# Attention output: every second product with v copied out of PSUM by ScalarE and its halves added by GpSimd

## The chip, the core and the metric

The kernel runs on one core of a Trainium2 chip. The core has four engines that compute: TensorE (PE in the profile; matrix products into PSUM), VectorE (DVE), ScalarE (ACT) and GpSimd (POOL). SyncE (SP) starts most of the transfers from and to HBM. Each engine works through its own list of instructions in order, and waits on counters (semaphores) that the other engines raise. The metric is the time in microseconds from the first to the last instruction of one execution and what lies around it; lower is better.

## The reference

Attention with a mask by clusters, over 2 x 8 = 16 heads of 768 rows and 64 columns, and two layers after it over the 1536 rows that come out:

```
mask   = argmax(q_n @ c_n.T)[:, None] == argmax(k_n @ c_n.T)[None, :]      # per head, 16 centroids
scores = where(mask, q @ k.T / 8, -1e9)
attn   = softmax(scores)
x      = attn @ v                      # 16 heads, put side by side: 1536 x 512
h      = x @ w_in                      # 1536 x 2048
g      = (a0 + a1 h + a2 h^2 + a3 h^3) / (1 + |b0||h| + |b1|h^2 + 1e-6)
x      = g @ w_out                     # 1536 x 512
out    = (silu(x @ w_gate) * (x @ w_val)) @ w_out2
```

Everything is float32. The kernel gets this precision from TensorE by splitting each operand into a high and a low part, and adding the products of the parts.

## The kernel before

The attention is written as a list of steps, and every engine runs the same list. A step holds the work of several tiles at different stages. A tile is 128 query rows of one head against its 768 keys, so a head has six tiles and there are 96. At step s:

- TensorE computes the scores of tile s (lines 1226 and 1229), turns the finished probabilities of tile s-5 (six transposes, line 1239, into PSUM banks 4 and 5, in two halves of three), and then makes a third of a product with v (lines 1254 and 1256). It also has the small products that find the clusters of a later head: the transposes of line 1278 and the product of line 1292 in two neighbouring steps of a head, and line 1313 in the next two.
- ScalarE takes the exponential of tile s-1 (line 811), and copies the transposed probabilities of tile s-5 out of PSUM, rounded to the high part, in two halves (line 829).
- VectorE takes the row maximum of tile s (line 1035), and subtracts the high part of tile s-5 from what stands in PSUM, again in two halves, which gives the low part (line 1057). TensorE may write the next tile's transposes into those two banks only after that: the first three wait for the first half of the subtraction of the tile before, the second three for its second half (lines 1236 to 1238).
- GpSimd divides three finished tiles by their row sums every third step (line 589). TensorE transposes them after that. It splits q, k and v of later heads (lines 597 to 617), parts of the first layer's weights (lines 624 and 626), and x (lines 636 and 638).

A product with v is made per group. A group is half a head, that is three tiles or 384 query columns, and there are 32 of them, numbered g. The high and the low part of v stand side by side as weights. So of the result in bank 6 (O_BANK) 64 partitions hold the product with the high part, and the other 64 that with the low part; for every second head the two are swapped by choosing r = 0 or 64, so that two heads fill the 128 partitions of x. The two have to be added. Before the change this is done in the step in which the product ends, last on both engines: ScalarE copies one half to x_part (line 839), and VectorE adds the other, straight from PSUM, to give x_raw (line 1066). TensorE begins the next group's product in the next step, after its transposes, and waits there for that addition (line 1251). When a pair of heads is complete, GpSimd waits for the additions and splits x into x_hi and x_lo.

Below, the steps of a head are counted 0 to 5. The product of an even group (g = 0, 2, ...) ends in step 4, that of an odd group in step 1. Step 4 is also the one in which line 1278 stands on TensorE, behind the product with v; line 1292 is in step 5, and line 1313 in steps 0 and 1. GpSimd has the split of a pair of heads at the end of its step 0, in every second head. Heads are numbered h = 0 to 15, and h holds groups 2h and 2h+1; h odd has r = 64.

After the last tile TensorE goes on without a pause with the first layer, in units n of 12 + 12 products of 512 columns, in which GpSimd multiplies once (line 516).

Of the kernel before, what the change touches and what calls it, by code (L numbers as in the profile page):

```python
# [21 lines left out]
def build_program(nc, q, k, v, centroids, w_in, w_out1, a, b, w_gate, w_val, w_out2, out):  # L22
# [44 lines left out]
    def at(name, shape, dt, offset):  # L67
        return nc.alloc_sbuf_tensor_at(name, shape, dt, offset=offset)
# [17 lines left out]
    x_lo = at("x_lo", [P, DC, NTOK], F32R, X_AT + X_BYTES)  # L86

    x_raw = at("x_raw", [P, DC, NTOK], F32, X_AT + X_BYTES)

# [125 lines left out]
    def sem(name):  # L215
# [4 lines left out]
    s_v_in = [sem(f"s_v_in{i}") for i in range(2)]  # L220
    s_vhi, s_vlo, s_logit_lo, s_logit_sum, s_xpart, s_xsum = (sem(x) for x in (
        "s_vhi", "s_vlo", "s_logit_lo", "s_logit_sum", "s_xpart", "s_xsum"))
    s_copy = [sem(f"s_copy{i}") for i in range(3)]
# [14 lines left out]
    s_pT, s_pT_hi, s_pT_lo, s_pv, s_xhi, s_xlo = (sem(x) for x in (  # L238
        "s_pT", "s_pT_hi", "s_pT_lo", "s_pv", "s_xhi", "s_xlo"))
    s_w1p_hi, s_w1p, s_w1hi, s_w1lo = (sem(x) for x in ("s_w1p_hi", "s_w1p", "s_w1hi", "s_w1lo"))  # L240
    s_w2sum, s_w2hi, s_w2lo, s_wohi, s_wolo = (sem(x) for x in (
# [122 lines left out]
    with block:  # L364
# [114 lines left out]
        def _(pool):  # L479
# [103 lines left out]
            for step in STEPS:  # L583
# [47 lines left out]
                if third == HALF - 1 and g1 % 4 == 3:  # L631
                    pool.wait_ge(s_xsum, g1 + 1)
                    finish_last()
                    h = g1 // 2
                    xh, xl, raw = x_pair(x_hi, h), x_pair(x_lo, h), x_pair(x_raw, h)
                    did(g.tensor_scalar(xh, raw, 1.0, 1.0, ALU.mult, ALU.mult), s_xhi)
                    pool.wait_ge(s_xhi, h // 2 + 1)
                    did(g.tensor_tensor(xl, raw, xh.bitcast(F32), ALU.subtract), s_xlo)
                    finish_last()
# [18 lines left out]
        def _(sc):  # L658
# [144 lines left out]
            for step in STEPS:  # L803
# [30 lines left out]
                if third == HALF - 1:  # L834
                    r = (g // 2) % 2 * D
                    sc.wait_ge(s_pv, g + 1)
                    if g:
                        sc.wait_ge(s_xsum, g)
                    s.activation(x_part[r:r + D, :], ps[D - r:P - r, O_BANK, 0:HC], ACT.Copy
                                 ).then_inc(s_xpart, 1)  # L840
                if head_at(step, S_CEN) == 0:
# [32 lines left out]
        def _(ve):  # L874
# [136 lines left out]
            for step in STEPS:  # L1011
# [49 lines left out]
                g, third = pv_at(step)  # L1061
                if third == HALF - 1:

                    ve.wait_ge(s_xpart, g + 1)
                    r = (g // 2) % 2 * D
                    v_.tensor_tensor(x_of(x_raw, g), ps[r:r + D, O_BANK, 0:HC],
                                     x_part[r:r + D, :], ALU.add).then_inc(s_xsum, 1)
# [31 lines left out]
        def _(pe):  # L1099
# [40 lines left out]
            def first_result(n):  # L1140
                u = n % NF1
                pe.wait_ge(s_glo, n + 1)
                if n == 0:
                    pe.wait_ge(s_pT_lo, 2 * NT)
                    pe.wait_ge(s_xsum, NG)
                for d in range(DC):
                    if u == 0 and n:
                        pe.wait_ge(s_yraw, (n // NF1 - 1) * DC + d + 1)
                    w = slice(DM + d * P, DM + (d + 1) * P)
                    last = three(ps[:, RES + d, :], w1_hi[u][:, w], w1_lo[u][:, w], g_hi[n % 3][:, :],  # L1150
                                 g_lo[n % 3][:, :], u == 0, u == NF1 - 1)
                last.then_inc(s_y, 1)
# [57 lines left out]
            for step in STEPS:  # L1210
# [33 lines left out]
                if g is not None:  # L1244

                    h = g // 2
                    if third == 0:
                        pe.wait_ge(s_pT_lo, T * (g + 1))
                        pe.wait_ge(s_vlo, h + 1)
                        if g:  # L1250
                            pe.wait_ge(s_xsum, g)
                    for kt in (2 * third, 2 * third + 1):
# [124 lines left out]
```

## Time and profile before

| | |
|---|---|
| three timed runs | 794.4, 795.75 and 795.83 us, median 795.75 |
| the profiled execution's own time | 794.28 us |
| its span, first to last instruction | 792.5 us |
| TensorE busy | 781.2 us (99%) |
| VectorE busy | 571.9 us (72%) |
| GpSimd busy | 522.7 us (66%) |
| ScalarE busy | 517.3 us (65%) |
| granted TensorE clock, mean | 0.996 |

The span is the time from the first to the last instruction of one execution that the hardware profiler took. The attention steps lie from about 20 to 262 us of it, and the two layers after that. A timeline row gives the start, the duration, the engine, the line, what is written and read, and the number of instructions merged into the row; the brackets give the idle time of the engine just before, and what ended it. Short gaps have no bracket. Ends of products on TensorE are modelled: each row of them looks longer than the time until the next one starts, so starts are compared here and not ends.

### The profile page before, as it was taken

The page shows a single profiled execution, that of the slowest core. Times are in us where ns is not written, and L with a number is a line of the kernel's source. Part 1 is how long each engine was busy: PE and PEld are TensorE (multiplying, and loading weights), DVE is VectorE, ACT ScalarE, POOL GpSimd, SP SyncE. Part 2 cuts the span into 40 slices and gives each one's busy share as a digit, 9 for nine tenths or more (in the row PEclk, how much of TensorE's full clock was granted, in tenths as well). Part 3 has the DMA queues.
Part 4 walks back from the last instruction along what each step waited for, and adds up shares of the span by engine and source line. Part 5 has one row for each costly group of instructions (what it writes and reads, how often), then busy time and mean ns, then how long its engine had stood idle before and what let it go on. Part 6 is the DMA issues. An engine that isn't in the chain of part 4 may idle for free.

```text
span 792.5 us, 12617 instructions
## 1 busy us (share of the span) xinstructions
PE 781.2 (99%) x4204; PEld 697.7 (88%) x4204; DVE 571.9 (72%) x1043; ACT 517.3 (65%) x957; POOL 522.7 (66%) x457
## 2 busy tenths in 40 slices
PE   8999999999999999999999999999999999999998
PEld 7799999999998888888888888899999999999997
DVE  5899999999997888778777777745445545554453
ACT  4888888888887787777767889744444444333322
POOL 4767988998575799322222288888889876655620
PEclk8999999999999999999999999999999999999999
DMA  8776555454310700000000011241111114111102
GB/s 206 180 199 162 143 140 125 116 145 121 85 60 19 221 28 0 1 1 1 1 1 0 1 55 54 66 147 50 32 54 53 37 45 134 54 28 53 28 1 80
DMA packets 57681, 57.92 MB, mean 73 GB/s; under 512 B 6608, under 2 KB 44304, under 8 KB 57616
## 3 DMA queue, kind: packets, MB, share of 16 engines
q1 hardware_dynamic: 57376, 56.52, 26.6%
q8 instruction: 34, 0.56, 0.3%
q10 hardware_dynamic: 240, 0.59, 0.3%
q14 instruction: 31, 0.25, 0.1%
HBM read 33.59 MB, written 3.15 MB: 46 GB/s over the span
## 4 chain that ended last, share of the span: by engine, by line
PE 87%; DVE 8%; issue 2%; ACT 2%; DMA 0%; DVEq 0%; ACTq 0%
PE ps L1111 18%; PE ps L1109 18%; PE ps L1110 18%; PE ps L1239 6%; PE ps L1204 4%; PE ps L1205 4%; PE ps L1203 4%; DVE neg_max L1035 3%; DVE probT_lo L1057 3%; PE ps L1254 3%; PE ps L1226 3%; PE ps L1256 3%; PE ps L1313 2%; PE ps L1229 2%; ACT prob L811 1%
## 5 line engine op out<-in xcount | busy, mean ns | idle before, releaser
L516 POOL TENSOR_TENSOR den<-den,mag 128x512 f32<-128x512 f32 x48 | 62.3, 1298 | 121.8 <-ACT den L689 121.6
L1111 PE MATMUL ps<-x_hi,w_lo 128*128 128x512 f32 (+1 forms) x384 | 139.5, 363 | 0.0
L1109 PE MATMUL ps<-x_hi,w_hi 128*128 128x512 f32 (+1 forms) x384 | 139.4, 363 | 0.0
L1110 PE MATMUL ps<-x_lo,w_hi 128*128 128x512 f32 (+1 forms) x384 | 139.3, 363 | 0.0
L575 POOL TENSOR_TENSOR w_lo<-w_raw,w_hi 128x768 fp32r<-128x768 f32 (+1 forms) x48 | 101.6, 2125 | 56.4 <-ACT w_hi L742 56.4
L589 POOL TENSOR_SCALAR prob<-prob,row_inv 128x768 f32<-128x768 f32 x96 | 85.6, 907 | 39.2 <-DVE row_inv L1049 38.7
L829 ACT ACTIVATE probT_hi<-ps 128x384 fp32r<-128x384 f32 x192 | 84.2, 489 | 25.9 <-PE ps L1239 24.2
L1057 DVE TENSOR_TENSOR probT_lo<-ps,probT_hi 128x384 fp32r<-128x384 f32 x192 | 96.8, 545 | 5.3 <-ACT probT_hi L829 4.0
L1035 DVE TENSOR_REDUCE neg_max<-ps 128x1 f32<-128x768 f32 x96 | 91.1, 950 | 8.8 <-PE ps L1229 8.5
L811 ACT ACTIVATE prob<-ps,neg_max 128x768 f32<-128x768 f32 x96 | 86.8, 905 | 10.8 <-DVE neg_max L1035 10.1
L1239 PE MATMUL ps<-ident,prob 128*128 128x128 f32 x576 | 81.7, 277 | 4.4 <-DVE probT_lo L1057 4.1
L1239 PEld LDWEIGHTS ps<-ident,prob 128*128 128x128 f32 x576 | 65.6, 140 | 17.0 <-issue 9.9
L1109 PEld LDWEIGHTS ps<-x_hi,w_hi 128*128 128x128 f32 x384 | 72.1, 188 | 8.2
L1110 PEld LDWEIGHTS ps<-x_lo,w_hi 128*128 128x128 f32 x384 | 72.1, 188 | 8.2
L1111 PEld LDWEIGHTS ps<-x_hi,w_lo 128*128 128x128 f32 x384 | 72.1, 188 | 7.5
L1111 PE MATMUL ps<-g_hi,w_lo 128*128 128x512 f32 x192 | 74.8, 390 | 0.0
L1110 PE MATMUL ps<-g_lo,w_hi 128*128 128x512 f32 x192 | 74.8, 390 | 0.0
L1109 PE MATMUL ps<-g_hi,w_hi 128*128 128x512 f32 x192 | 74.8, 390 | 0.0
L1254 PE MATMUL ps<-probT_hi,v_split 128*128 128x384 f32 x192 | 72.5, 378 | 0.0
L763 ACT ACTIVATE act_hi<-ps 128x384 fp32r<-128x384 f32 x48 | 23.6, 492 | 64.6 <-DVE ps L992 43.7
L1256 PE MATMUL ps<-probT_lo,v_split 128*128 128x384 f32 x192 | 64.6, 337 | 0.0
L959 DVE TENSOR_TENSOR sum<-ps,gate 128x384 f32<-128x384 f32 x24 | 13.4, 557 | 68.9 <-PE ps L1111 68.9
(145 smaller groups left out, 1987.5 us busy)
## 6 DMA issues: line engine op xcount, KB each, us to landing
k_hihi<-qk_hi SPq DMA_DIRECT2D x32, 192.0 KB, 4.0
w_raw<-in_moe_w_gate SPq DMA_DIRECT2D x48, 128.0 KB, 2.3
w_raw<-in_moe_w_val SPq DMA_DIRECT2D x48, 128.0 KB, 2.5
w_raw<-in_moe_w_in SPq DMA_DIRECT2D x16, 256.0 KB, 3.7
w_raw<-in_moe_w_out SPq DMA_DIRECT2D x16, 256.0 KB, 5.0
qk_raw<-in_q SPq DMA_DIRECT2D x16, 192.0 KB, 3.4
q_hilo<-qk_hi SPq DMA_DIRECT2D x16, 192.0 KB, 3.4
qk_low<-qk_hi SPq DMA_DIRECT2D x16, 192.0 KB, 4.5
```

What stands on the lines that cost most here:

```text
L575: did(g.tensor_tensor(lo[:, wave, :], raw[:, wave, :], hi[:, wave, :].bitcast(F32), ALU.subtract), s_w2lo)
L589: did(g.tensor_scalar(prob[i][:, :], prob[i][:, :], row_inv[:, i:i + 1], 1.0, ALU.mult, ALU.mult), s_norm)
L811: s.activation(prob[i % T][:, :].rearrange("p (c n) -> p c n", c=2), ps[:, bank:bank + 2, 0:HC], ACT.Exp, bias=neg_max[:, i % T:i % T + 1] ...
L829: s.activation(probT_hi[g % 2][:, n * HALF:(n + 1) * HALF, c:c + P], ps[:, PT_BANK + n, 0:HC].rearrange("p (k n) -> p k n", k=HALF), ACT.C ...
L1035: v_.tensor_reduce(neg_max[:, i % T:i % T + 1], ps[:, bank:bank + 2, 0:HC], AX.XY, ALU.max, negate=True).then_inc(s_max, 1)
L1057: v_.tensor_tensor(probT_lo[g % 2][:, keys, c:c + P], ps[:, PT_BANK + n, 0:HC].rearrange("p (k n) -> p k n", k=HALF), probT_hi[g % 2][:, k ...
L1109: mm(dst, hi, m_hi, start=start, stop=False)
L1110: mm(dst, hi, m_lo, start=False, stop=False)
L1111: return mm(dst, lo, m_hi, start=False, stop=stop)
L1239: last = transpose(ps[:, PT_BANK + n, kt % HALF * P:(kt % HALF + 1) * P], prob[i % T][:, kt * P:(kt + 1) * P], ident[:, :])
L1254: mm(ps[:, O_BANK, 0:HC], vv, probT_hi[g % 2][:, kt, :], start=(kt == 0), stop=False)
L1256: last = mm(ps[:, O_BANK, 0:HC], vv, probT_lo[g % 2][:, kt, :], start=False, stop=(kt == T - 1))
```

## The change

The groups with an even number take another way out of PSUM. ScalarE makes two copies, one of each half: the first straight to x_low, a new name for the memory in which x_hi will stand later, the second to x_raw. VectorE does nothing for these groups. TensorE waits for the second copy (s_xmain) before the next product. When GpSimd splits a pair of heads, it first adds the two for the even groups of both heads in one instruction, 128 partitions by 384 columns, waits for that, and then splits as before. Odd groups go as they did, with counters that count half as far.

```diff
+    x_low = at("x_low", [P, DC, NTOK], F32, X_AT)
...
                 if third == HALF - 1 and g1 % 4 == 3:
-                    pool.wait_ge(s_xsum, g1 + 1)
+                    h = g1 // 2
+                    pool.wait_ge(s_xmain, h + 1)
+                    pool.wait_ge(s_xsum, h + 1)
                     finish_last()
-                    h = g1 // 2
                     xh, xl, raw = x_pair(x_hi, h), x_pair(x_lo, h), x_pair(x_raw, h)
+                    did(g.tensor_tensor(raw[:, 0:HC], raw[:, 0:HC], x_pair(x_low, h)[:, 0:HC], ALU.add), s_xboth)
+                    finish_last()
                     did(g.tensor_scalar(xh, raw, 1.0, 1.0, ALU.mult, ALU.mult), s_xhi)
...
                     sc.wait_ge(s_pv, g + 1)
-                    if g:
-                        sc.wait_ge(s_xsum, g)
-                    s.activation(x_part[r:r + D, :], ps[D - r:P - r, O_BANK, 0:HC], ACT.Copy
-                                 ).then_inc(s_xpart, 1)
+                    if g % 2:
+                        if g > 1:
+                            sc.wait_ge(s_xsum, g // 2)
+                        s.activation(x_part[r:r + D, :], ps[D - r:P - r, O_BANK, 0:HC], ACT.Copy
+                                     ).then_inc(s_xpart, 1)
+                    else:
+                        s.activation(x_of(x_low, g), ps[D - r:P - r, O_BANK, 0:HC], ACT.Copy)
+                        s.activation(x_of(x_raw, g), ps[r:r + D, O_BANK, 0:HC], ACT.Copy).then_inc(s_xmain, 1)
...
-                if third == HALF - 1:
-
-                    ve.wait_ge(s_xpart, g + 1)
+                if third == HALF - 1 and g % 2:
+
+                    ve.wait_ge(s_xpart, g // 2 + 1)
...
                 if n == 0:
                     pe.wait_ge(s_pT_lo, 2 * NT)
-                    pe.wait_ge(s_xsum, NG)
+                    pe.wait_ge(s_xsum, NH)
...
                         if g:
-                            pe.wait_ge(s_xsum, g)
+                            pe.wait_ge(s_xmain if g % 2 else s_xsum, (g + 1) // 2)
```

The order of ScalarE's instructions in head 9, from step 4 to the step 0 that follows, before (line 829 copies the transposes, 811 is the exponential, 819 belongs to the clusters):

```order
L829 ACTIVATE probT_hi_206<-ps 128x3x128 x2
L839 ACTIVATE x_part<-ps 64x384
L811 ACTIVATE prob_201,row_sum<-ps,neg_max 128x768
L819 ACTIVATE topT<-ps 96x256
L829 ACTIVATE probT_hi_205<-ps 128x3x128 x2
L811 ACTIVATE prob_202,row_sum<-ps,neg_max 128x768
```

The same place on ScalarE after the change (the lines and the buffer numbers are shifted; 816, 824 and 834 are the former 811, 819 and 829):

```order
L834 ACTIVATE probT_hi_207<-ps 128x3x128 x2
L848 ACTIVATE x_low<-ps 64x384
L849 ACTIVATE x_raw<-ps 64x384
L816 ACTIVATE prob_202,row_sum<-ps,neg_max 128x768
L824 ACTIVATE topT<-ps 96x256
L834 ACTIVATE probT_hi_206<-ps 128x3x128 x2
L816 ACTIVATE prob_203,row_sum<-ps,neg_max 128x768
```

One copy of 64x384 has become two, and both stand ahead of the exponential, the cluster copy and the next tile's copies of the transposes.

VectorE's order at the same place of head 9, before, around the addition of line 1066 (1035 is the row maximum, 1057 the low part):

```order
L1035 TENSOR_REDUCE neg_max<-ps 128x1
L1057 TENSOR_TENSOR probT_lo_213<-ps,probT_hi_206 128x3x128 x2
L1066 TENSOR_TENSOR x_raw<-ps,x_part 64x384
L1035 TENSOR_REDUCE neg_max<-ps 128x1
L1057 TENSOR_TENSOR probT_lo_212<-ps,probT_hi_205 128x3x128 x2
```

VectorE's order there after the change (1044 and 1066 are the former 1035 and 1057):

```order
L1044 TENSOR_REDUCE neg_max<-ps 128x1
L1066 TENSOR_TENSOR probT_lo_214<-ps,probT_hi_207 128x3x128 x2
L1044 TENSOR_REDUCE neg_max<-ps 128x1
L1066 TENSOR_TENSOR probT_lo_213<-ps,probT_hi_206 128x3x128 x2
L1033 TENSOR_SCALAR clusterT<-ps 96x128
```

The addition is gone from between the low part of one tile and the row maximum of the next; nothing has moved into its place.

GpSimd's order where a pair of heads is split, before:

```order
L606 TENSOR_TENSOR qk_lo_186<-qk_raw_183,qk_hi_189 128x768
L636 TENSOR_SCALAR x_hi<-x_raw 128x768
L638 TENSOR_TENSOR x_lo<-x_raw,x_hi 128x768
L589 TENSOR_SCALAR prob_197<-prob_197,row_inv 128x768
L589 TENSOR_SCALAR prob_198<-prob_198,row_inv 128x768
```

And after:

```order
L608 TENSOR_TENSOR qk_lo_187<-qk_raw_184,qk_hi_190 128x768
L639 TENSOR_TENSOR x_raw<-x_raw,x_low 128x384
L641 TENSOR_SCALAR x_hi<-x_raw 128x768
L643 TENSOR_TENSOR x_lo<-x_raw,x_hi 128x768
L591 TENSOR_SCALAR prob_198<-prob_198,row_inv 128x768
L591 TENSOR_SCALAR prob_199<-prob_199,row_inv 128x768
```

The new addition stands ahead of the split, and so also ahead of the divisions of the next three tiles.

## Rows read from the trace of the kernel before

**Rows 1.** Busy time in 36:264 us: length, then each engine with its instructions.

```profile
36.00:264.00 228.00, 223.95 (x1493) 208.50 (x1492) 210.85 (x433) 189.54 (x424) 181.75 (x181) 1.00 0.47 120
```

**Rows 2.** Waits of TensorE in 36:264: total us, times, longest.

```profile
PE ps L1239 <- DVE probT_lo L1057: 3.9, 13, 0.5
```

**Rows 3.** Timeline of TensorE, head 9, step 4, to head 10, step 4.

```profile
168.00 0.92 PE L1239 MATMUL ps<-ident,prob 128*128 128x128 f32 x6 [0.22 <-DVE probT_lo L1057]
...
170.37 0.82 PE L1239 MATMUL ps<-ident,prob 128*128 128x128 f32 x6
171.11 0.41 PE L1254 MATMUL ps<-probT_hi,v_split 128*128 128x384 f32 x1
...
172.70 0.91 PE L1239 MATMUL ps<-ident,prob 128*128 128x128 f32 x6
173.37 0.42 PE L1254 MATMUL ps<-probT_hi,v_split 128*128 128x384 f32 x1
...
178.25 0.82 PE L1239 MATMUL ps<-ident,prob 128*128 128x128 f32 x6
178.83 0.42 PE L1254 MATMUL ps<-probT_hi,v_split 128*128 128x384 f32 x1
...
182.86 0.92 PE L1239 MATMUL ps<-ident,prob 128*128 128x128 f32 x6 [0.34 <-DVE probT_lo L1057]
```

**Rows 4.** Timeline of ScalarE, head 9, steps 4 and 5, and the next step 0.

```profile
169.65 0.48 ACT L839 ACTIVATE x_part<-ps 64x384 f32<-64x384 f32 x1 [0.21 <-PE ps L1256]
170.16 0.91 ACT L811 ACTIVATE prob<-ps,neg_max 128x768 f32<-128x768 f32 x1
...
171.31 0.86 ACT L829 ACTIVATE probT_hi<-ps 128x384 fp32r<-128x384 f32 x2
...
173.24 0.89 ACT L829 ACTIVATE probT_hi<-ps 128x384 fp32r<-128x384 f32 x2 [0.20 <-PE ps L1239]
```

**Rows 5.** Timeline of VectorE, head 9, steps 4 and 5.

```profile
169.36 1.01 DVE L1057 TENSOR_TENSOR probT_lo<-ps,probT_hi 128x384 fp32r<-128x384 f32 x2
170.40 0.56 DVE L1066 TENSOR_TENSOR x_raw<-ps,x_part 64x384 f32<-64x384 f32 x1
170.99 0.96 DVE L1035 TENSOR_REDUCE neg_max<-ps 128x1 f32<-128x768 f32 x1
171.98 1.02 DVE L1057 TENSOR_TENSOR probT_lo<-ps,probT_hi 128x384 fp32r<-128x384 f32 x2
```

**Rows 6.** Timeline of all engines, head 12, steps 4, 5 and 0.

```profile
213.97 0.49 ACT L839 ACTIVATE x_part<-ps 64x384 f32<-64x384 f32 x1 [0.21 <-PE ps L1256]
...
215.64 0.86 ACT L829 ACTIVATE probT_hi<-ps 128x384 fp32r<-128x384 f32 x2
...
216.15 1.02 DVE L1057 TENSOR_TENSOR probT_lo<-ps,probT_hi 128x384 fp32r<-128x384 f32 x2
...
216.90 0.88 PE L1239 MATMUL ps<-ident,prob 128*128 128x128 f32 x6
...
217.53 0.42 PE L1254 MATMUL ps<-probT_hi,v_split 128*128 128x384 f32 x1
```

**Rows 7.** Timeline of GpSimd, head 9, the split of x and after.

```profile
167.10 1.83 POOL L638 TENSOR_TENSOR x_lo<-x_raw,x_hi 128x768 fp32r<-128x768 f32 x1
169.03 2.68 POOL L589 TENSOR_SCALAR prob<-prob,row_inv 128x768 f32<-128x768 f32 x3
...
172.27 1.01 POOL L617 TENSOR_TENSOR v_split<-v_raw,v_split 128x384 fp32r<-128x384 f32 x1
...
176.77 2.66 POOL L589 TENSOR_SCALAR prob<-prob,row_inv 128x768 f32<-128x768 f32 x3
```

**Rows 8.** Timeline of ScalarE and VectorE, head 13, step 5.

```profile
228.73 0.86 ACT L829 ACTIVATE probT_hi<-ps 128x384 fp32r<-128x384 f32 x2
229.43 1.02 DVE L1057 TENSOR_TENSOR probT_lo<-ps,probT_hi 128x384 fp32r<-128x384 f32 x2
```

**Rows 9.** Timeline of GpSimd in the first layer, behind the last split of x.

```profile
270.34 1.30 POOL L516 TENSOR_TENSOR den<-den,mag 128x512 f32<-128x512 f32 x1 [2.84 <-ACT den L689]
```

More of the change, by code:

```diff
@@ L220, in build_program @@
     s_v_in = [sem(f"s_v_in{i}") for i in range(2)]
-    s_vhi, s_vlo, s_logit_lo, s_logit_sum, s_xpart, s_xsum = (sem(x) for x in (
-        "s_vhi", "s_vlo", "s_logit_lo", "s_logit_sum", "s_xpart", "s_xsum"))
+    s_vhi, s_vlo, s_logit_lo, s_logit_sum, s_xpart, s_xsum, s_xmain = (sem(x) for x in (
+        "s_vhi", "s_vlo", "s_logit_lo", "s_logit_sum", "s_xpart", "s_xsum", "s_xmain"))
     s_copy = [sem(f"s_copy{i}") for i in range(3)]
@@ L239, in build_program @@
         "s_pT", "s_pT_hi", "s_pT_lo", "s_pv", "s_xhi", "s_xlo"))
+    s_xboth = sem("s_xboth")
     s_w1p_hi, s_w1p, s_w1hi, s_w1lo = (sem(x) for x in ("s_w1p_hi", "s_w1p", "s_w1hi", "s_w1lo"))
```

## Prediction, made before the changed kernel was run

> **What bounds the kernel now.** I read the busy time of the attention stretch first, then TensorE's waits there, then the timeline of one head engine by engine. TensorE looks busy for 223.95 of 228 us, VectorE for 210.85, ScalarE for 189.54, GpSimd for 181.75 [rows 1]. So TensorE sets the pace, VectorE is close behind it, and ScalarE has some 2.4 us free in each of 16 heads. The sums alone speak for the change: they move work from the second busiest engine to two that have room. Whether it is so depends on which engine ends the wait at each place, so I follow head 9, whose even group ends in step 4.
>
> TensorE's only recorded waits are for VectorE's low parts: 3.9 us in 13 places [rows 2]. More are hidden in the starts. Six transposes that nothing stops are followed by the product with v 0.58 us after their start (178.25 to 178.83). The six of step 5 take 0.74 (170.37 to 171.11) and those of step 0 0.67 (172.70 to 173.37) [rows 3]. The 0.16 of step 5 is the wait for VectorE's addition for the even group, which ends at 170.40 + 0.56 = 170.96 [rows 5]. The 0.09 of step 0 is the second three transposes waiting for the second half of tile 5's low part, which ends at 171.98 + 1.02 = 173.00 [rows 5]. (By tile 5 I mean the one transposed in step 5.) The largest wait is in step 4 (0.34 recorded at 182.86) [rows 3]. It comes from VectorE's run of steps 2 and 3, which does not hold the even group's addition: that one comes after the wait, not before it. So the change cannot remove it.
>
> What matters is what the low part of tile 5 waited for. In head 9 the row maximum ended at 170.99 + 0.96 = 171.95 and the low part began at 171.98, so VectorE was last there, and the removed addition stood ahead of it [rows 5]. But ScalarE is right behind: it began its copies of tile 5 at 171.31 [rows 4]. In head 12 the low part began at 216.15, 0.51 behind ScalarE's copies at 215.64 [rows 6], which are 0.43 each (0.86 for two). There ScalarE is already last. By that 0.51, head 9 would have allowed 171.82: VectorE was last by only 0.16.
>
> **The change, part by part.** *ScalarE, 16 more copies.* A copy is 0.48, and from its start to that of the exponential behind it 0.51 pass (169.65 to 170.16) [rows 4]. It started when TensorE's product ended, after an idle 0.21, so it cannot start sooner. All that follows it in the list moves: the exponential, the cluster copy and the copies of tile 5. For heads with r = 64 I take 0.51 for the second copy. For r = 0 the second copy reads and writes the same partitions, as the pair of line 829 does, two of which cover 0.86, so 0.43 each; I take 0.40 to 0.51, and use 0.40. Bounds for both: 0.37 (0.86 less one copy of 0.49) and 0.51.
>
> *VectorE, 16 fewer additions* of 0.56, 9.0 us of busy time. Behind the removed one the row maximum waits for scores that TensorE finished shortly after 170.37; VectorE would be ready at about 171.5 instead of 171.95. It then waits for ScalarE.
>
> *Together, r = 64.* Tile 5's copies start at 171.31 + 0.51 = 171.82, its low part at 171.82 + 0.51 = 172.33 instead of 171.98: 0.35 later, I use 0.36. The transposes of step 0 need it, so the product with v behind them moves from 173.37 to 173.73. TensorE does gain the 0.16 in step 5, but meets the later low part in step 0 and waits there: the gain is inside the 0.36. *r = 0.* The low part was bound by ScalarE already, so it moves by the full 0.40, and 217.53 becomes 217.93 [rows 6]. Nothing takes this back in the head: from step 0 to step 2 TensorE runs without waits, and the wait of step 4 follows from VectorE's work on the scores of step 2, which are as late.
>
> *GpSimd, 8 additions of 128x384.* The same operation on the same shape took 1.01 [rows 7], and waits for it to finish cost some 0.08 (the 167.10 + 1.83 = 168.93 to 169.03 behind the split is such a wait, 0.10). So 1.09 each. Bounds: 0.9, and 1.4 since two reads of x at this place are new. Behind it stand the divisions of the next three tiles. In head 9 they start at 169.03; one is 2.68 / 3 = 0.89, so the first is done at 169.92 and TensorE turns that tile at 170.37 [rows 3, 7]. With about 0.13 for the signal, 0.32 us are free, and 1.09 are added: the transposes of step 5 start at 171.14, 0.77 late. ScalarE's copies follow the start of the transposes by 0.54 (172.70 to 173.24) [rows 3, 4], so they could start at 171.68, still before the 171.82 at which ScalarE is free, so the two delays lie side by side. TensorE itself does not recover all of it. From the product of step 5 to the transposes of step 0 are 172.70 - 171.11 = 1.59, so those start at 171.14 + 0.58 + 1.59 = 173.31 and the product behind them at 173.89. That is 0.52 late instead of 0.36; I use 0.50. GpSimd's list brings the split at this place in every second head; I count heads 5, 7, 9 and 11 so, and head 3, the first, with those that only have ScalarE's delay (if not, 0.14 more). The later divisions of step 0, at 176.77 for a tile turned at 178.25, have 0.46 free and get 1.09 more against TensorE's own 0.50: about 0.13 is missing there, but the wait of step 4 follows from the scores and absorbs it. Nothing is charged; if it is not absorbed, 0.5 us in all.
>
> *The last heads.* Head 13 has no clusters to find; the low part starts at 229.43 and ScalarE's copies at 228.73 [rows 8], so 228.73 + 0.51 + 0.51 = 229.75, 0.32 later. Head 14 is like the r = 0 heads, 0.40. In head 15 TensorE works on the first layer meanwhile, nothing. Behind the last split the first layer's multiplication on GpSimd is 1.09 late, once; the one behind it had 2.84 of idle time ahead [rows 9], so nothing is carried on. It is 0, or at most 1.09.
>
> *The sum.* 8 heads of r = 0 at 0.40 = 3.2; heads 5, 7, 9, 11 at 0.50 = 2.0; heads 1 and 3 at 0.36 = 0.7; head 13 at 0.32 = 0.3: +6.2 us. After the attention TensorE is never idle for long, so all of it reaches the end. The profiled execution's own 794.28 (span 792.5) becomes 800.5. That execution was faster than the three timed runs; the middle of all four is 795.1, and the median of the three 795.75. I forecast 801.0 us, between 800.5 and 802.0.
>
> The trace has ScalarE's copy to x_part at 0.48 and no overlap with what follows it. The Trainium skill, "ScalarE: Activation LUTs", section "What ACT_TABLE_LOAD costs", gives 186 ns + 0.833 ns for each column, which is 506 ns as an estimate for 384, and says that back-to-back ACTIVATEs overlap by about 93 ns. The row shows the duration nearly so and the overlap not; the pair of line 829 shows it. By the page each copy would add 0.41, and two overlapping ones 0.31 over the one of today; the sum would come to about +4.9 and the time to 799.2.
>
> **The rivals.** *VectorE's relief decides.* If the second copy were hidden, or if VectorE's lists and not ScalarE's set tile 5, the waits would go: 0.16 + 0.09 in 7 heads of r = 64 and 0.05 in 8 others, 2.2 us, and one addition of 0.56 each in heads 13 and 14, where VectorE hardly idles: 3.3 in all, 791.0. For it: the busy sums. Against: the 0.51 in head 12, and only 0.16 in head 9. It decides if the copies of tile 5 start less than 0.16 later than now in the r = 64 heads.
>
> *GpSimd decides.* The new addition takes 1.4 rather than 1.09, or the late divisions of step 0 are not absorbed. Then heads 5, 7, 9 and 11 lose 0.31 more for the first and 0.13 + 0.31 for the second, 3.0 together; with 0.51 for every copy another 0.9, so +10, 804.4. It starts to count once the divisions are over 0.32 late, which they are.
>
> *The copies are short.* At 0.37 for each of the two, 0.74 instead of 0.51, r = 0 heads lose 0.23, heads 1 and 3 0.23 - 0.16 = 0.07, head 13 nothing, and those with GpSimd keep 0.50: 1.8 + 0.1 + 2.0 = +4.0, 798.3. For it: the pair of line 829. Against: nothing overlaps the copy to x_part now.
>
> *Nothing to see.* The loss per head is 0.1 or less because TensorE's gain in step 5 counts after all: +1.5 or less.
>
> **Chances.** The forecast 0.60, GpSimd decides 0.12, short copies 0.15: these three, 0.87, are slower. Nothing to see 0.07, VectorE's relief 0.06. A measurement of this kernel can tell a change from about 0.2%, 1.6 us. The range is 797.0 to 804.0: its lower end is 1.3 below the short copies, for a term of GpSimd's that is smaller than I make it, and its upper end is just under the GpSimd case.
>
> **What would show it.** Right: ScalarE has two rows of 64x384 in step 4 and the exponential 0.9 to 1.0 behind the start of the first. VectorE's low part of tile 5 begins 0.5 behind ScalarE's copies in every head, with an idle time of 0.4 to 0.8 that names ScalarE. TensorE's transposes of step 0 wait for the low part. A head takes 15.1 to 15.3 us instead of 14.86 (168.00 to 182.86). Busy time falls by 9 on VectorE and grows by 7.8 on ScalarE and 8.1 on GpSimd. In heads 5, 7, 9 and 11 TensorE's transposes of step 5 wait for GpSimd's divisions. Wrong: if the start of the exponential moves by under 0.2, or the low part still begins when the row maximum ends, the first step of the argument fails; if heads take 14.7 us or less, the second.

## The result, and the profile after the change

| | before | after |
|---|---|---|
| median, timed on the same chip | 795.08 us (794.18 to 795.84, 6 runs) | 800.47 us (799.47 to 803.22, 6 runs) |
| the profiled execution | 794.28 us | 800.42 us |
| its span | 792.5 us | 798.6 us |

The ratio is 1.0076, with a 95% interval of 1.0054 to 1.0097: slower, by 4.3 to 7.7 us. The forecast was 801.0. The medians differ by 5.4 us and the two profiled executions by 6.1; the prediction's own sum was 6.2.

The first view is the busy time of the whole span on the page of the kernel after, the second its busy time in 36 to 264 us, which answers to [rows 1] (PE, PEld, DVE, ACT, POOL, then clock, share of the DMA engines and GB/s).

```profile
PE 784.4 (98%) x4204; PEld 696.8 (87%) x4204; DVE 563.9 (71%) x1027; ACT 523.6 (66%) x973; POOL 530.6 (66%) x465
```

```profile
36.00:264.00 228.00, 221.04 (x1465) 202.76 (x1464) 199.63 (x412) 191.40 (x433) 183.40 (x184) 1.00 0.46 116
```

VectorE has 8.0 us less in the span, ScalarE 6.3 more and GpSimd 7.9 more. So the change does what it says, and the sums of busy time look better balanced than before. TensorE, which sets the pace, is the one that lost: 221.04 of 228 us busy where it was 223.95.

The waits in 36 to 264 us (total, times, longest) name the two causes. VectorE's low part waited for ScalarE 5 times before, 4.0 us in all; now it is 18 times and 14.5 us. TensorE's recorded wait for VectorE is about that of [rows 2], and waits for GpSimd's divisions are new (PEld is the weight load ahead of the same transposes). New as well is a wait of the cluster product of line 1301 (1292 before) for ScalarE's cluster copy, which the second copy delays too.

```profile
DVE probT_lo L1066 <- ACT probT_hi L834: 14.5, 18, 1.8
...
PEld ps L1248 <- POOL prob L591: 4.9, 9, 0.9
...
PE ps L1248 <- DVE probT_lo L1066: 4.0, 13, 0.9
...
PE ps L1248 <- POOL prob L591: 2.6, 5, 0.6
...
PEld ps L1301 <- ACT topT L824: 2.2, 8, 0.4
```

Now head 9, engine by engine. TensorE, answering to [rows 3] (all of after is 3.62 us later at the first of these rows, for what the nine heads before it lost):

```profile
171.62 0.92 PE L1248 MATMUL ps<-ident,prob 128*128 128x128 f32 x6 [0.21 <-DVE probT_lo L1066]
...
174.71 0.88 PE L1248 MATMUL ps<-ident,prob 128*128 128x128 f32 x6 [0.56 <-POOL prob L591]
175.34 0.42 PE L1263 MATMUL ps<-probT_hi,v_split 128*128 128x384 f32 x1
...
176.95 0.82 PE L1248 MATMUL ps<-ident,prob 128*128 128x128 f32 x6
177.53 0.42 PE L1263 MATMUL ps<-probT_hi,v_split 128*128 128x384 f32 x1
...
187.03 0.92 PE L1248 MATMUL ps<-ident,prob 128*128 128x128 f32 x6 [0.28 <-DVE probT_lo L1066]
```

A head is the distance between the first row and the last: 15.41 us, against 14.86. ScalarE, answering to [rows 4], and below them the same copies of head 10 (r = 0):

```profile
173.27 0.48 ACT L848 ACTIVATE x_low<-ps 64x384 f32<-64x384 f32 x1 [0.21 <-PE ps L1265]
173.77 0.48 ACT L849 ACTIVATE x_raw<-ps 64x384 f32<-64x384 f32 x1
174.28 0.90 ACT L816 ACTIVATE prob<-ps,neg_max 128x768 f32<-128x768 f32 x1
...
175.43 0.86 ACT L834 ACTIVATE probT_hi<-ps 128x384 fp32r<-128x384 f32 x2
...
188.69 0.49 ACT L848 ACTIVATE x_low<-ps 64x384 f32<-64x384 f32 x1 [0.21 <-PE ps L1265]
189.19 0.49 ACT L849 ACTIVATE x_raw<-ps 64x384 f32<-64x384 f32 x1
189.57 0.88 ACT L816 ACTIVATE prob<-ps,neg_max 128x768 f32<-128x768 f32 x1
```

The exponential stands 1.01 us behind the start of the first copy in head 9 and 0.88 in head 10, where one copy had 0.51 before. VectorE, answering to [rows 5], and GpSimd, answering to [rows 7]:

```profile
174.19 0.96 DVE L1044 TENSOR_REDUCE neg_max<-ps 128x1 f32<-128x768 f32 x1 [0.20 <-PE ps L1238]
175.94 1.02 DVE L1066 TENSOR_TENSOR probT_lo<-ps,probT_hi 128x384 fp32r<-128x384 f32 x2 [0.80 <-ACT probT_hi L834]
```

```profile
169.80 1.00 POOL L639 TENSOR_TENSOR x_raw<-x_raw,x_low 128x384 f32<-128x384 f32 x1
170.89 0.83 POOL L641 TENSOR_SCALAR x_hi<-x_raw 128x768 fp32r<-128x768 f32 x1
171.80 1.84 POOL L643 TENSOR_TENSOR x_lo<-x_raw,x_hi 128x768 fp32r<-128x768 f32 x1
173.75 2.68 POOL L591 TENSOR_SCALAR prob<-prob,row_inv 128x768 f32<-128x768 f32 x3
```

VectorE finished the row maximum at 175.15 and then idled 0.80 for ScalarE's copies: the 0.56 that was taken off it has turned into idle time. GpSimd's new addition takes 1.09 from its start to that of the split, and the divisions, and TensorE's transposes at 174.71, stand behind all three.

ScalarE and VectorE in heads 12 and 13, answering to [rows 6, 8]: in both the low part again begins 0.51 behind ScalarE's copies, and it now waits for them.

```profile
221.08 0.85 ACT L834 ACTIVATE probT_hi<-ps 128x384 fp32r<-128x384 f32 x2
...
221.59 1.02 DVE L1066 TENSOR_TENSOR probT_lo<-ps,probT_hi 128x384 fp32r<-128x384 f32 x2 [0.66 <-ACT probT_hi L834]
...
234.66 0.86 ACT L834 ACTIVATE probT_hi<-ps 128x384 fp32r<-128x384 f32 x2
...
235.17 1.02 DVE L1066 TENSOR_TENSOR probT_lo<-ps,probT_hi 128x384 fp32r<-128x384 f32 x2 [0.75 <-ACT probT_hi L834]
```

TensorE's transposes of step 0 then wait for the first half of that low part. The wait is recorded only where little else fills the time, as in head 14, which has no clusters to find. Before, and below it after:

```profile
243.05 0.92 PE L1239 MATMUL ps<-ident,prob 128*128 128x128 f32 x6 [0.47 <-DVE probT_lo L1057]
```

```profile
248.45 1.02 DVE L1066 TENSOR_TENSOR probT_lo<-ps,probT_hi 128x384 fp32r<-128x384 f32 x2 [0.61 <-ACT probT_hi L834]
...
249.15 0.92 PE L1248 MATMUL ps<-ident,prob 128*128 128x128 f32 x6 [0.91 <-DVE probT_lo L1066]
```

The transposes start 0.70 behind the low part here, and 0.71 behind it in head 10 (191.22 and 191.93). Head 14 loses 0.37 like the other heads with r = 0, though it has no cluster product. So the late low part is enough to explain the loss, and the late cluster copy lies beside it.

In the first layer GpSimd still idles 2.84 ahead of its second multiplication, as in [rows 9], so the addition ahead of the last split carries nothing on:

```profile
277.53 1.29 POOL L518 TENSOR_TENSOR den<-den,mag 128x512 f32<-128x512 f32 x1 [2.84 <-ACT den L694]
```

To see where the 6.1 us were lost I took, in every trace, the start of TensorE's transposes of step 4 of each head, and how much further it lies from the kernel before's than one head earlier. This is the loss caused by that head. After the change it is 0.34 to 0.38 in the heads with r = 0, 0.34 and 0.37 in heads 1 and 3, 0.54 to 0.57 in heads 5, 7, 9 and 11, and 0.31 in head 13. The sum is 6.1, and none of it comes back in the two layers.

### The profile page after: what moved, and what is told of

Its sections match the earlier page's. It is cut to its first block, busy times and chain, and to the rows that moved or that the text cites. A ratio compares the mean times of both kernels' runs of the same rounds, so it can differ in the third digit from the quotient of the medians.

```text
span 798.6 us, 12609 instructions
## 1 busy us (share of the span) xinstructions
PE 784.4 (98%) x4204; PEld 696.8 (87%) x4204; DVE 563.9 (71%) x1027; ACT 523.6 (66%) x973; POOL 530.6 (66%) x465
## 4 chain that ended last, share of the span: by engine, by line
PE 83%; POOL 7%; DVE 4%; ACT 3%; issue 2%; DMA 0%; POOLq 0%; ACTq 0%; DVEq 0%
PE ps L1118 18%; PE ps L1120 18%; PE ps L1119 18%; PE ps L1248 5%; PE ps L1213 4%; PE ps L1214 4%; PE ps L1212 4%; POOL prob L591 2%; PE ps L1263 2%; PE ps L1265 2%; PE ps L1235 2%; DVE neg_max L1044 2%; PE ps L1238 2%; PE ps L1322 2%; DVE probT_lo L1066 1%
## 5 line engine op out<-in xcount | busy, mean ns | idle before, releaser
L1066 DVE TENSOR_TENSOR probT_lo<-ps,probT_hi 128x384 fp32r<-128x384 f32 x192 | 96.7, 545 | 14.8 <-ACT probT_hi L834 14.5
```

Of the source, the lines that this page charges most:

```text
L1066: v_.tensor_tensor(probT_lo[g % 2][:, keys, c:c + P], ps[:, PT_BANK + n, 0:HC].rearrange("p (k n) -> p k n", k=HALF), probT_hi[g % 2][:, k ...
```

## The experiments

The same reading for every kernel. "Ratio" is to the kernel before, run on the same chip. The two columns of heads are means of the loss of a head. "Sum" is that of heads 2 to 14: in heads 0 and 1 the start of the program still plays in.

| kernel | ratio (95%) | heads 4, 6, 8, 10, mean | heads 5, 7, 9, 11, mean | sum, us |
|---|---|---|---|---|
| the change | 1.0076 (1.0054 to 1.0097) | 0.36 | 0.55 | 5.4 |
| a, GpSimd's addition alone | 1.0012 (1.0001 to 1.0023) | 0.0 | 0.35 | 1.6 |
| b, one more copy on ScalarE alone | 1.0076 (1.0059 to 1.0093) | 0.42 | 0.40 | 5.4 |
| c, VectorE's relief, one ScalarE copy as before | 0.9969 (0.9957 to 0.9982) | -0.07 | -0.14 | -1.6 |
| d, the change without GpSimd's addition | 1.0062 (1.0040 to 1.0084) | 0.36 | 0.35 | 4.6 |
| f, the odd groups instead | 1.0041 (1.0027 to 1.0055) | 0.10 | 0.49 | 3.5 |
| v1, before, row sums later | 0.9994 (0.9984 to 1.0005) | -0.05 | 0.22 | 0.6 |
| v2, the change, row sums later | 1.0125 (1.0112 to 1.0138) | 0.10 | 1.46 | 10.1 |
| v4, c with row sums later | 0.9970 (0.9957 to 0.9982) | -0.28 | 0.29 | -0.8 |
| g, the change, x split in step 3 | 1.0062 (1.0046 to 1.0078) | 0.36 | 0.36 | 4.5 |
| h, g with later row sums in step 3 | 1.0058 (1.0043 to 1.0072) | 0.10 | 0.11 | 3.1 |
| w, one copy of 128 partitions | 0.9963 (0.9949 to 0.9977) | -0.10 | -0.23 | -1.9 |
| w late, w with later row sums in step 3 | 0.9961 (0.9947 to 0.9974) | -0.27 | -0.42 | -1.2 |

My theory: ScalarE's second copy delays every head by some 0.35, GpSimd's addition the heads with a split of x by a little more, and VectorE's relief does not count because ScalarE is last there. The rivals: GpSimd is the main cause, or VectorE's relief is worth more than I make it.

**The parts one by one.** a adds to the kernel before one GpSimd addition where the change has it (its result is not used), b one ScalarE copy behind that of the even groups (of a constant, not used).

```diff
+                    did(g.tensor_tensor(x_pair(x_low, h)[:, 0:HC], raw[:, 0:HC], raw[:, 0:HC], ALU.add), s_xboth)
+                    finish_last()
...
+                    if g % 2 == 0:
+                        s.activation(x_of(x_low, g).rearrange("p (c n) -> p c n", c=HALF),
+                                     ident[:, :].unsqueeze(1).to_broadcast([P, HALF, P])[r:r + D],
+                                     ACT.Copy).then_inc(s_xmain, 1)
```

> The kernel before, with one extra GpSimd addition of 128x384 ahead of each split of x (its result is not used). Theory (ScalarE's second copy costs about 0.35 in every head, GpSimd's addition lies beside it and shows only where the divisions stand behind a split): alone, GpSimd makes TensorE's transposes of step 5 about 0.77 late in heads 5, 7, 9 and 11, of which 0.5 stays, and nothing elsewhere: +2.1 us. Rival (GpSimd's addition is what costs in the changed kernel): +5 or more, spread over all heads. Rival (GpSimd is always covered): under 0.5.

> The kernel before, with one extra ScalarE copy of 64x384 (from a constant in SBUF, result not used) behind the copy to x_part of every even group; VectorE adds as before, GpSimd as before. Theory: +5.3 us, 0.35 in each of 15 heads, because what VectorE saves in the changed kernel is worth nothing. Rival (VectorE's relief is worth something there, and hides part of the copy's price): clearly more than the changed kernel without its GpSimd addition, +7 or more. [...]

One more copy on ScalarE alone costs as much as the whole change, 0.39 to 0.43 in every head but one; GpSimd's addition alone gives 1.6 us, and only in the heads whose split stands in front of divisions that are waited for. TensorE, step 5 of head 9 in a:

```profile
173.27 0.88 PE L1243 MATMUL ps<-ident,prob 128*128 128x128 f32 x6 [0.38 <-POOL prob L591]
```

a is a little too kind: its addition reads the same operand twice and took 0.83, the change's 1.01 (rows below and above), so the true one would cost about 0.35 + 0.18 = 0.53 in those heads. b is a little too harsh: its exponential starts 0.55 after the added copy in head 9, where the change has 0.51. So the two equal sums are partly chance: the change has 0.8 us from GpSimd in them, and b has none.

```profile
168.54 0.83 POOL L638 TENSOR_TENSOR x_low<-x_raw 128x384 f32<-128x384 f32 x1
```

```profile
175.39 0.53 ACT L845 ACTIVATE x_low<-ident 64x384 f32<-64x384 f32 x1
175.94 0.91 ACT L814 ACTIVATE prob<-ps,neg_max 128x768 f32<-128x768 f32 x1
```

d is the change without GpSimd's addition, c that and without the first of the two copies (both, and v4 below, leave one of the two halves of the even groups out of x).

```diff
-                    did(g.tensor_tensor(raw[:, 0:HC], raw[:, 0:HC], x_pair(x_low, h)[:, 0:HC], ALU.add), s_xboth)
-                    finish_last()
...
-                        s.activation(x_of(x_low, g), ps[D - r:P - r, O_BANK, 0:HC], ACT.Copy)
```

> The changed kernel without GpSimd's addition, so x lacks the second half of v's split in the even groups. Theory: the four heads that lost 0.55 lose 0.35 like the others: 0.8 us less than the changed kernel, +5.3 over the one before. Rival (GpSimd decides): back to within 2 us of the kernel before.

> The changed kernel without GpSimd's addition and without the first of the two copies, so ScalarE makes one copy in each group as before and VectorE adds in odd groups alone (x lacks one half of the split v in the even groups). It is the relief of VectorE by itself. Theory: ScalarE's chain is last or 0.16 behind, so heads with r = 64 gain some 0.1 each and the others nothing: -0.5 to -1.0 us against the kernel before. Rival (VectorE decides): -3.3 us.

d shows the two causes side by side: without GpSimd's addition heads 5, 7, 9 and 11 lose 0.35 like the others, so the addition costs 0.20 on top in each of four heads. It would be 0.53 on its own, but 0.35 of that ScalarE loses anyway. c has the relief, and one copy on ScalarE as before. It gained 1.6 us in heads 2 to 14 (1.4 to 3.4 us by its ratio), where I had said 0.5 to 1.0, but not all of it is VectorE's. In the heads with r = 64 the low part now begins 0.51 behind ScalarE's copies instead of 0.67, and they gain 0.14, near the 0.16 that the prediction read there: 0.9 us in heads 3 to 13. In the heads with r = 0 the low part stood 0.51 behind ScalarE before and still does; there c's copy reads and writes partitions from 0, where x_part's read from 64, and the exponential follows it after 0.39 instead of 0.51. ScalarE being last there, this shorter copy is the likely source of their 0.7 us. (Head 0 lost 0.81 and head 1 0.16 in c: TensorE's first scores of a later head waited for the transfer of its cluster rows, which landed at 38.61 and 53.53, each 0.06 before the weights were loaded.) With one copy on ScalarE the low part of tile 5 in c still waits 0.30 for ScalarE (head 9), so it is not the 3.3 of the rival:

```profile
170.17 0.86 ACT L832 ACTIVATE probT_hi<-ps 128x384 fp32r<-128x384 f32 x2
```

```profile
169.42 0.96 DVE L1041 TENSOR_REDUCE neg_max<-ps 128x1 f32<-128x768 f32 x1 [0.20 <-PE ps L1235]
170.68 1.02 DVE L1063 TENSOR_TENSOR probT_lo<-ps,probT_hi 128x384 fp32r<-128x384 f32 x2 [0.30 <-ACT probT_hi L832]
```

**The same on the odd groups.** Their product ends in step 1, between copies of transposes ahead of which ScalarE has idle time. f swaps the two kinds of group: GpSimd adds the other half of the columns, and TensorE's waits are swapped to match, one more before the first layer. This is ScalarE of the change around that place, in head 10:

```profile
180.21 0.88 ACT L834 ACTIVATE probT_hi<-ps 128x384 fp32r<-128x384 f32 x2 [0.96 <-PE ps L1248]
181.24 0.48 ACT L845 ACTIVATE x_part<-ps 64x384 f32<-64x384 f32 x1 [0.15 <-PE ps L1265]
...
183.01 0.87 ACT L834 ACTIVATE probT_hi<-ps 128x384 fp32r<-128x384 f32 x2 [0.27 <-PE ps L1248]
```

```diff
-                    if g % 2:
+                    if g % 2 == 0:
...
-                if third == HALF - 1 and g % 2:
+                if third == HALF - 1 and g % 2 == 0:
```

> The changed kernel with the parts swapped: odd groups leave by two ScalarE copies and GpSimd's addition (the other half of the columns), even groups by one copy and VectorE's addition. The counts of all instructions are those of the changed kernel; only the step differs (1 instead of 4). Theory (the place decides): in step 1 ScalarE has idle time behind the copy, so the next tile's low part moves by 0.15 in heads with r = 64 and 0.05 in the others, 1.6 us, and GpSimd's addition costs the 1.6 it costs alone: +3.2 us against the kernel before, half of the changed one. Rival (the amount of ScalarE's work decides): +6, as in the changed kernel.

In heads 6, 8 and 10, where only ScalarE has more to do, the loss is 0.03 to 0.05: the same two copies cost nearly nothing in the place where they meet idle time. In heads 7, 9 and 11 it is 0.55 to 0.57, close to the 0.53 estimated from a for GpSimd's addition by itself, and TensorE's transposes of step 5 wait for the divisions (0.52 in head 9). So it is the place and not the work that costs. (Head 4 lost 0.28 because TensorE waited 0.32 for a transfer: the cluster rows of a later head landed at 100.54, and its weights were loaded at 100.60. Head 5 lost 0.28 and heads 12 and 13 0.38 and 0.29; I did not follow these.)

**Can VectorE's time be bought back?** Its row sums (lines 1046 and 1049 of before) stand ahead of a low part that TensorE waits for in step 4. In v1, v2 and v4 the low part goes ahead of them.

```diff
                                      ALU.max, negate=True).then_inc(s_max, 1)
+                i = tile_at(step - LAG)
+                if i is not None:
...
+                                         ALU.subtract).then_inc(s_pT_lo, 1)
                 if (step - HALF) % HALF == 0 and 0 <= (step - HALF) // HALF < NG:
```

> The kernel before, with VectorE's sum and reciprocal of the row sums moved from ahead of the low parts to behind them in steps 0 and 3 (0.28 us less ahead of the wait of step 4). Theory: the transposes of step 4 start 0.27 earlier, but VectorE's list up to the low part of tile 5 is as long as before and holds the addition of the even group, so heads with r = 64 give it all back; those with r = 0 keep 0.1: -1 us or less. Rival (the wait of step 4 is worth its 0.27 in every head): -4 us.

> The changed kernel with the same move of VectorE's row sums. Theory: here VectorE has lost the even group's addition and ScalarE's chain, which begins with TensorE's product of step 4, is last; starting it 0.27 earlier gains 0.25 in most heads: -3.5 us against the changed kernel, +2.5 against the one before. So the same edit is worth three times as much as in the kernel before. Rival (VectorE's relief is worth nothing in any order): -1 us as there.

> The kernel in which VectorE is relieved and ScalarE makes one copy per group (x lacks one half of the split v in the even groups), with the same move of the row sums. It bounds what the relief could bring if its price on ScalarE and GpSimd were nothing. Theory: -1.8 from the relief and 0.25 more per head: -5.5 us against the kernel before.

In heads without a split it did about what I expected in v2 and v4, 0.26 and 0.21 less (0.36 to 0.10, -0.07 to -0.28), and 0.05 less in v1. In the others it went wrong, most in v2, so that v2 lost 10.1 us where I had said 2.5, and v4 gained 0.8 (1.4 to 3.4 by its ratio) where I had said 5.5: I had not followed the row sums to GpSimd, whose divisions need them. GpSimd and TensorE in v2, head 3:

```profile
80.40 1.01 POOL L639 TENSOR_TENSOR x_raw<-x_raw,x_low 128x384 f32<-128x384 f32 x1
...
82.42 1.83 POOL L643 TENSOR_TENSOR x_lo<-x_raw,x_hi 128x768 fp32r<-128x768 f32 x1
84.35 2.68 POOL L591 TENSOR_SCALAR prob<-prob,row_inv 128x768 f32<-128x768 f32 x3
...
85.31 1.19 PE L1248 MATMUL ps<-ident,prob 128*128 128x128 f32 x6 [1.74 <-POOL prob L591]
```

Later divisions push all that stands behind them on GpSimd, the splits of q and k, the addition and the split of x, and the next divisions last: TensorE waited 1.74. So GpSimd, harmless in most heads of the change, becomes the bound when the row sums ahead of its chain are moved.

**GpSimd's split earlier.** g puts the addition and the split of x at the end of step 3, where GpSimd idles before its divisions; h has the later row sums beside it, in step 3 alone.

```diff
-    X_STEP, LAST_X_STEP = 5, 2
+    X_STEP, LAST_X_STEP = 2, 2
```

> The change as it is, but GpSimd adds and splits x at the end of step 3 instead of the end of step 0: there it idled about 2.1 us before the next divisions. My theory (a delay of ScalarE's 0.35 us in every head, and 0.2 more in heads 5, 7, 9 and 11 from GpSimd's addition ahead of the divisions): those four heads lose 0.35 like the others, so +5.3 us against the kernel before, ratio about 1.0066, 0.8 less than the change. Rival, that the addition of GpSimd costs wherever it stands (its buffer traffic slows others): the four heads keep 0.55, ratio 1.0077.

> As the run with the earlier split, and VectorE's row sums in step 3 stand behind the low parts instead of ahead of them. If the move did harm before only because GpSimd's divisions stood behind the split and then behind the row sums too, it now gives what it gave in heads without the split, 0.25 in each: 0.10 lost per head, +1.5 us against the kernel before, ratio 1.002. Rival, that the later row sums hold the divisions up by themselves: over 0.35 per head, ratio above 1.007.

g came out as expected: 0.36 in heads 5, 7, 9 and 11, and the same GpSimd work costs nothing in another place. In h the row sums now give their 0.25 in all eight heads of the table. But heads 2 and 12 lost 0.73 and 0.77, and the sum is 3.1 where I had said 1.5: in head 12 the divisions behind the split of x came late again, and TensorE waited for them. h's ratio is no better than g's within the intervals.

```profile
226.75 0.88 PE L1261 MATMUL ps<-ident,prob 128*128 128x128 f32 x6 [0.37 <-POOL prob L591]
```

**Without the second copy.** One ScalarE copy of all 128 partitions takes the even group out of PSUM. Three transfers (DMAs) for each pair of heads, of 96 KB each, then bring the halves to the partitions where GpSimd adds them, in step 3 as in g.

```diff
-    X_STEP, LAST_X_STEP = 5, 2
+    X_STEP, LAST_X_STEP = 2, 2
...
+    def both(h):
+
+        return x_pair(x_low, h)[:, HC:S] if h % 2 else x_pair(x_raw, h)[:, 0:HC]
...
+            def move_x(h):
+                sp.wait_ge(s_xmain, h + 1)
+                low, src, moved = x_pair(x_low, h), both(h), s_xmove[h // 2 % 2]
+                if h % 2:
+                    sp.wait_ge(moved, 48 * (h // 4) + 16)
+                    sp.dma_start(x_pair(x_raw, h)[D:P, 0:HC], src[D:P, :]).then_inc(moved, 16)
+                    sp.dma_start(low[D:P, 0:HC], src[0:D, :]).then_inc(moved, 16)
+                else:
+                    sp.dma_start(low[0:D, 0:HC], src[D:P, :]).then_inc(moved, 16)
...
-                    pool.wait_ge(s_xmain, h + 1)
+                    pool.wait_ge(s_xmove[h // 2 % 2], 48 * (h // 4 + 1))
...
-                        s.activation(x_of(x_low, g), ps[D - r:P - r, O_BANK, 0:HC], ACT.Copy)
-                        s.activation(x_of(x_raw, g), ps[r:r + D, O_BANK, 0:HC], ACT.Copy).then_inc(s_xmain, 1)
+                        s.activation(both(g // 2), ps[:, O_BANK, 0:HC], ACT.Copy).then_inc(s_xmain, 1)
```

> The even groups leave PSUM by one ScalarE copy of 128 partitions instead of two of 64; three DMAs per pair of heads put the halves onto the right partitions, and GpSimd adds them, at the end of step 3. ScalarE then has as many copies as before the change, VectorE 16 additions fewer. My theory: as with VectorE's relief alone, 0.14 less in the heads with r=64 and 0.07 in the others, -1.8 us against the kernel before, ratio 0.998. Rivals: the DMAs bring x late for the split, which would show as a wait of GpSimd and of the divisions behind it, +0.2 or more in every second head, ratio 1.000 or above; or a copy of 128 partitions takes longer than one of 64 (0.48), then about 0.3 in each head, ratio above 1.004.

> The run with one copy of 128 partitions, and VectorE's row sums of step 3 behind the low parts. With the split of x out of the way of the divisions the gain of 0.28 that the heads without a split showed should hold in all: -4.0 to -4.5 us against the kernel before, ratio about 0.9945. Rival: the divisions wait for the row sums and take it back, 0 to -2 us, ratio 0.998 to 1.000.

w took 791.93 us (791.42 to 793.95), before it 795.79: a ratio of 0.9963, faster than both kernels, and its interval ends just below the 0.998 that I expected. Its ScalarE in head 9, and VectorE's low part of tile 5:

```profile
170.55 0.49 ACT L868 ACTIVATE x_low<-ps 128x384 f32<-128x384 f32 x1 [0.21 <-PE ps L1284]
170.94 0.90 ACT L836 ACTIVATE prob<-ps,neg_max 128x768 f32<-128x768 f32 x1
...
172.08 0.86 ACT L854 ACTIVATE probT_hi<-ps 128x384 fp32r<-128x384 f32 x2
```

```profile
172.60 1.02 DVE L1085 TENSOR_TENSOR probT_lo<-ps,probT_hi 128x384 fp32r<-128x384 f32 x2 [0.18 <-ACT probT_hi L854]
```

The copy of 128 partitions is as long as one of 64, and in this head the exponential follows it after 0.39, where it was 0.51 in [rows 4]. That 0.12 fits the 0.09 that w has over c in the heads with r = 64 (-0.23 against -0.14). GpSimd waits for no DMA, and TensorE for no division, so the rival with late transfers did not come about as I had put it. But in head 3, which lost 0.17, TensorE's first scores of a later head waited 0.41, and 1.16 in w late, which lost 0.75 there. TensorE's weight loads in w and in w late:

```profile
85.14 0.30 PEld L1254 LDWEIGHTS ps<-k_hihi,q_hilo 128*128 128x128 f32 x2 [0.41 <-issue]
```

```profile
85.62 0.30 PEld L1267 LDWEIGHTS ps<-k_hihi,q_hilo 128*128 128x128 f32 x2 [1.16 <-issue]
```

The kernel waits there for the cluster rows of that head, which come through the same queue as the new transfers. The last of them landed at 85.08 in w and at 85.56 in w late, each 0.06 before the weights were loaded; in the kernel before they had landed at 80.76 and the weights were loaded at 83.47. How much of the delay is owed to the new transfers is not shown: c and f, which do not have them, met the same wait in other heads.

w late missed its expectation of -4.0 to -4.5 us. It gained 0.27 and 0.42 in the heads that the table shows, but lost 0.48, 0.75 and 0.77 in heads 2, 3 and 12. In heads 2 and 12 it is again the chain on GpSimd that ends with the divisions; this is its TensorE in head 12:

```profile
221.40 0.88 PE L1280 MATMUL ps<-ident,prob 128*128 128x128 f32 x6 [0.86 <-POOL prob L611]
```

Its sum is no better than w's. Giving up the later row sums in those three heads alone was not tried.

## Why the prediction was right, step by step

*ScalarE's second copy delays what is behind it.* Right. In head 9 (r = 64) the two copies cover 1.01, where I had 0.51 twice. In head 10 (r = 0) they cover 0.88, 0.37 more than the one of before, where I used 0.40. The sign was 0.9 to 1.0 for both. b shows that a second copy costs this much by itself.

*The low part of tile 5 follows ScalarE by 0.51.* Right: 175.43 to 175.94, and in head 9 all of it was predicted within 0.01 (171.82 and 172.33, plus the 3.62 of the heads before). VectorE idled 0.80 ahead of it. In all of heads 0 to 14 the low part begins 0.51 or 0.52 behind ScalarE's copies, with 0.61 to 0.81 of idle time ahead, and the transposes of step 0 wait for it, as the signs said.

*The loss per head.* For r = 0 I had 0.40, and 0.34 to 0.38 was measured; 8 such heads make 0.4 us less. The copy's delay of 0.37 is the difference: it lies at the lower of my two bounds. For heads 1 and 3 I had 0.36, measured 0.34 and 0.37. Head 13: 0.32 against 0.31.

*GpSimd.* I predicted the transposes of step 5 in head 9 at 171.14, which with the 3.62 is 174.76; they started at 174.71, named the divisions as their releaser, and step 0 came at 176.95 (predicted 176.93). No row gave the 0.13 that I took for the signal: the first division was done at 173.75 + 0.89 = 174.64, 0.07 before the transposes. The loss was 0.54 to 0.57 where I had 0.50, four times. That the later divisions of the same head are absorbed held too. d and g confirm that the addition is worth 0.20 in each of these heads and nothing elsewhere. So the sum's 6.2 against 6.1 is a little luck: 0.4 too much in the heads with r = 0 and 0.2 too little here. The forecast of 801.0 was put above that sum's 800.5 because the three timed runs had been slower than the profiled one. The medians then differed by 5.4 only, so that 801.0 came within 0.6 of the 800.47 is also a matter of where the runs fell.

*VectorE's relief counts for nothing.* Right in the change. By itself it is worth 0.14 in a head with r = 64, as c shows, for the 0.16 by which VectorE had been last. In the change it is hidden behind ScalarE: b, without the relief, loses 0.42 and 0.40 in a head, d, with it, 0.36 and 0.35, and of the difference of 0.05 to 0.06 some 0.04 to 0.05 is b's longer copy (the exponential stands 1.06 behind the first copy in b's head 9, against 1.01).

*The signs.* Busy time fell by 8.0 on VectorE where I had said 9, and grew by 7.9 on GpSimd (8.1) and by 6.3 on ScalarE, where I had said 7.8; the copies' own rows do sum to 7.8 more, and which other rows are shorter I did not trace. The head took 15.41, above the 15.1 to 15.3 that I gave; a head with r = 64 and the split is 14.86 + 0.55, and the range that I wrote fitted only the heads without GpSimd's part.

Of the Trainium skill's rule, "ScalarE: Activation LUTs", section "What ACT_TABLE_LOAD costs", that back-to-back ACTIVATEs overlap by about 93 ns: the trace agrees for some rows and not for others. 189.19 with 0.49 is followed at 189.57, an overlap of 0.11; 173.77 with 0.48 is followed at 174.28, none. The 799.2 that the prediction worked out from it lies 1.2 below the profiled 800.42.

## What to carry to other kernels

Balance of busy time says little: work moved off the second busiest engine cost 0.35 a head, because it landed on the engine that was last at that place, or only 0.16 behind the last. Ask of each place, not of each engine, who ends the wait; the same two copies cost 0.04 where ScalarE was idle, and the same GpSimd addition nothing three steps earlier. Here one copy over all 128 partitions at the price of 64, with three transfers for each pair of heads, beat a second instruction on a busy engine: a ratio of 0.9963 against g's 1.0062. But look at what else waits for that queue.

## What the runs showed of the hardware

- One ScalarE copy of 128x384 from PSUM takes 0.49, like one of 64x384 (0.48 to 0.49). The exponential starts 0.51 after one whose source or target begins at partition 64 (173.77 to 174.28), and 0.39 after one where both begin at 0 (189.19 to 189.57, and w's of 128 partitions). In c, where only r differs, it is 0.51 and 0.39 as well. The partitions are not all of it: in b's head 10 the copy from partition 64 to 0 is followed after 0.39 (190.16 to 190.55) by the copy of a constant in SBUF, and that one, with both at 0, after 0.53 by the exponential.
- GpSimd's addition of 128x384 took 1.01 with two operands and 0.83 when both were the same.
- The start of the program differs from run to run. In the profiled runs step 4 of head 0 lies between 1.3 us earlier and 2.5 us later than before's, with little or no change ahead of it. The granted TensorE clock at that time differs too: in 8 to 12 us it is 0.51 in g (0.52 in the kernel before), about the lower of its two levels (1.2 GHz), and 1.00 in w, the upper one (2.4 GHz), while TensorE was busy all the time in both. But it does not set the place of head 0: g has it 0.3 us earlier than the kernel before, and w 1.9 later. What does was not found. The runs of the kernel before fall into two clusters, at about 794.2 and 796.0 us. So kernels were compared head by head, where 0.05 us can be seen. The two stretches are shown below, g's and then w's (the clock is the third number from the end):

```profile
8.00:12.00 4.00, 4.00 (x19) 3.80 (x18) 1.56 (x4) 0.66 (x2) 3.26 (x3) 0.51 1.03 247
```

```profile
8.00:12.00 4.00, 4.00 (x19) 3.81 (x18) 2.02 (x4) 0.33 (x1) 2.80 (x3) 1.00 1.02 245
```
